# Sums of six weight blocks and of the third row group on VectorE instead of GpSimd, token numbers stored from on-chip rows, a new order of SyncE's transfers, and turn counts loaded at the top of a pair

## The chip, the cores and the metric

The program runs on one core of a Trainium2 chip. The metric is the device time of one execution in microseconds (us); lower is better. Profiles are single executions of the same program, taken by the hardware profiler. In the rows PE is TensorE, DVE VectorE, ACT ScalarE, POOL GpSimd and SP SyncE; an engine's name with a q (DVEq, SPq) is its sequencer, which runs register instructions and issues transfers.

## The reference

The reference chains three blocks on 2304 tokens (4 batches of 576) of width 512. All numbers are float32.

```python
# 1. attention with a feature map, 8 heads of 64; phi(x) = [exp(p), exp(-p)], p = x @ w_phi - max|x @ w_phi|
kv = einsum('bhsf,bhsd->bhfd', phi(k), v); z = sum_s phi(k)
x = (phi(q) @ kv) / (phi(q) @ z + 1e-6)                 # -> (2304, 512)
# 2. mixture of 8 experts, F = 1024, one expert per token
e_idx = argmax(x @ w_gate, axis=1); gate_w = softmax(x @ w_gate)[e_idx]; eom = sigmoid(x @ w_output_gate)
x[mask_e] = gate_w * eom[:, e] * (maximum(x[mask_e] @ w1[e], 0) @ w2[e])
# 3. gated feed-forward block, F = 1536, rms norm ahead of it
xn = x / sqrt(mean(x * x) + 1e-6) * rms_g
out = (silu(xn @ w_gate) * (xn @ w_val)) @ w_out
```

With these inputs three of the eight experts get tokens.

## The kernel before

**Numbers and products.** Each float32 operand of a large product is split into a high part in a reduced format (a copy by ScalarE, names ending in H) and a low remainder (a subtraction by VectorE, names ending in L); three matmuls, high by high, high by low and low by high, replace one. TensorE is busy nearly all the time, so the order of the other engines' work is written out by hand, one program per engine, with semaphores between them. `wait_ge` holds only the engine that issues it, and everything behind it in that engine's program.

**Routing.** Attention's rows, with the token's number in column DM (512) and its gate in column 513, are scattered to `xs_dram`, one region per expert. A table `tab` in SBUF holds, for the active experts in order ("turns"), how many steps each has (TILES), its first step (FIRST), its number, and for each step its row and output column. There are eight steps of 288 rows in this run, 0 to 7, in three turns: steps 0 and 1, steps 2 to 5, and steps 6 and 7. Step 0 is taken early, beside the end of attention. Every engine walks over the table by itself: `over_turns` (on VectorE `turns`) loops over pairs of turns, since weights are double-buffered; for each of the two turns of a pair `turn_of` (L417, L418) loads the number of steps and the first step into registers, and `If(tiles > 0)` skips an empty turn. The fourth turn, the second of the second pair, is empty here.

**A step** has eight chunks m = 0 to 7: hidden(m) and outputs(m - 2) on TensorE, relu and its high half on ScalarE, the low half hmL on VectorE. Beside them, SyncE loads the rows of a step into the one buffer `xin` (`rows_next`, once TensorE has transposed the previous rows, semaphore pe_XT), GpSimd multiplies them by their gates (`gate_rows`), TensorE transposes them at the end of the previous step (L1080), ScalarE copies the step's outputs to `x2g` in the next step's chunk 0 (`copy_out`, L1371; it needs the store of the rows before it to have landed, semaphore xst), GpSimd squares and adds them (`add_squares`), VectorE normalises them (`normal`, L1805), and SyncE stores them to `xn_dram` (`rows_out`). In the first step of a turn the next turn's weights are split, and GpSimd issues their loads (`raw_in`). Each step also prepares the weights of one of the final block's twelve visits: SyncE loads them (`step_weights_in`), VectorE adds (`weight_sums`, L1918 to L1926) and they are split and stored to `t_dram` (`weights_out`). `numbers_out` copies 288 token numbers from `xs_dram` to `ids_dram`, as a transfer of 288 elements of 4 bytes; the numbers are read back once, near the middle of the final block.

**The final block** multiplies by gate and value weights in 2x2 blocks by a scheme of seven products instead of eight, which needs sums of blocks on both sides. A unit is one visit v (128 of 1536 columns of gate and value) for one group sg of 768 rows: seven products of six matmuls each, L1207 to L1209. There are 36 units; UNITS orders them: units 0 to 2 are of group 0, units 3 to 5 of group 1, and group 2 first comes up in unit 10. A group's rows are loaded by `group_in` into `xst`; four sums per group (`row_sums`) go to `s_sum`; ScalarE and VectorE then make seven high and seven low halves. Sums of groups 0 and 2 are made by GpSimd (L863 to L869), of group 1 by VectorE in unit 1 (L2058 to L2068). Visits 6 to 11 (MADE) get their weights raw, and GpSimd makes their sums (`made_sums`, L851 to L855) ahead of MADE_AT; the other visits' operands come from `t_dram` (`operands_in`).

Within unit u VectorE does: first_gate(u), the work listed for position "A", second_gate(u - 1) (L2010, after TensorE's last product of unit u - 1), the work for "B", hidden_rows(u - 1) (L2024 and L2026, after ScalarE's sigmoid, L1482), values(u) (L2018). TensorE's fourth product in unit u + 1, `last_product(u)`, waits for values(u). ScalarE's sigmoid of unit u waits until the hidden rows of unit u - 2, which lie in the same buffer `hid`, are stored (`hidden_out` on SyncE, L640). The outputs follow from h_dram, after 720 us.

**SyncE's order** in the loop over steps and at the entry of the final block is that of its program:

```python
with e.Fori(0, total - 2) as n:
    rows_next(n + 2)          # waits for pe_XT
    weights_out(n + 1)        # waits for the step's split weights
    step_weights_in(n + 2)    # waits until that store has landed
    rows_out(n, col)          # waits for the normalised rows
    numbers_out(n, col, row)
```

## Time and profile before

| | us |
|---|---|
| median of three runs | 870.38 |
| lowest and highest | 868.96, 873.25 |
| the profiled execution, its time | 873.63 |
| its span in the trace | 871.9 |
| TensorE busy | 840.2 |
| VectorE busy | 538.9 |
| ScalarE busy | 347.3 |
| GpSimd busy | 161.4 |

The span is the time from the first to the last instruction of the trace; the profiled execution's own time is 1.7 us more. By stages, attention and step 0 take to 243 us, the steps 1 to 7 to 445 us, the 36 units to 720 us, and the outputs the rest. Matmuls are pipelined, so a matmul's duration is longer than the distance to the next one. A row of waits gives the engine and line that waited, the engine and tile it waited for, the total in us, the number of waits and the longest.

### The profile page before, as it was taken

The page shows a single profiled execution, that of the slowest core. Times are in us where ns is not written, and L with a number is a line of the kernel's source. Part 1 is how long each engine was busy: PE and PEld are TensorE (multiplying, and loading weights), DVE is VectorE, ACT ScalarE, POOL GpSimd, SP SyncE. Part 2 cuts the span into 40 slices and gives each one's busy share as a digit, 9 for nine tenths or more (in the row PEclk, how much of TensorE's full clock was granted, in tenths as well). Part 3 has the DMA queues.
Part 4 walks back from the last instruction along what each step waited for, and adds up shares of the span by engine and source line. Part 5 has one row for each costly group of instructions (what it writes and reads, how often), then busy time and mean ns, then how long its engine had stood idle before and what let it go on. Part 6 is the DMA issues. An engine that isn't in the chain of part 4 may idle for free.

```text
span 871.9 us, 16594 instructions
## 1 busy us (share of the span) xinstructions
PE 840.2 (96%) x6216; PEld 757.3 (87%) x6217; DVE 538.9 (62%) x934; ACT 347.3 (40%) x547; POOL 161.4 (19%) x169
## 2 busy tenths in 40 slices
PE   8999999998988999999989999999999999999997
PEld 6685867767988999999989999999999998888885
DVE  5688786989766954445569777666765774212210
ACT  4544454573155533322354443333433443212211
POOL 1010302112350433203421031111110000101101
PEclk9999999999999999999999999999999999999999
DMA  8613713112349544554662852232421945343320
GB/s 285 209 57 138 275 54 108 55 38 75 127 175 267 227 114 97 141 148 150 184 230 77 280 180 79 79 80 79 142 71 54 357 150 184 123 139 125 125 101 36
DMA packets 65226, 122.41 MB, mean 140 GB/s; under 512 B 9200, under 2 KB 43120, under 8 KB 62480
## 3 DMA queue, kind: packets, MB, share of 16 engines
q1 hardware_dynamic: 57600, 91.98, 34.3%
q0 software_dynamic: 3488, 17.85, 5.3%
q10 hardware_dynamic: 4080, 11.80, 3.9%
...
## 4 chain that ended last, share of the span: by engine, by line
PE 78%; DVE 11%; issue 6%; DMA 2%; ACT 1%; DVEq 1%; SPq 0%; another core or an unknown queue 0%; POOLq 0%; POOL 0%; ACTq 0%
PE ps L1207 9%; PE ps L1209 9%; PE ps L1208 9%; PE ps L1259 5%; PE ps L1258 5%; PE ps L1260 5%; PE ps L956 3%; PE ps L1115 3%; PE ps L1116 3%; PE ps L1117 3%; PE ps L1128 3%; PE ps L1130 3%; PE ps L1129 3%; PE ps L1011 3%; PE ps L916 2%
## 5 line engine op out<-in xcount | busy, mean ns | idle before, releaser
L1207 PE MATMUL ps<-sH,tb 128*128 128x384 f32 x504 | 171.0, 339 | 5.9 <-DVE val L2018 2.9
L1208 PE MATMUL ps<-sL,tb 128*128 128x384 f32 x504 | 170.0, 337 | 0.0
L1209 PE MATMUL ps<-sH,tb 128*128 128x384 f32 x504 | 169.9, 337 | 0.0
L1207 PEld LDWEIGHTS ps<-sH,tb 128*128 128x128 f32 x504 | 95.0, 189 | 8.5 <-DVE val L2018 4.9
L1208 PEld LDWEIGHTS ps<-sL,tb 128*128 128x128 f32 x504 | 95.1, 189 | 0.1
L1209 PEld LDWEIGHTS ps<-sH,tb 128*128 128x128 f32 x504 | 95.2, 189 | 0.0
L2036 DVE TENSOR_TENSOR hTL<-h_st,hTH 128x768 fp32r<-128x768 f32 x36 | 33.0, 954 | 97.4 <-ACT hTH L1516 97.4
L1260 PE MATMUL ps<-woH,hTL 128*128 128x512 f32 x216 | 84.1, 389 | 0.0
L1259 PE MATMUL ps<-woL,hTH 128*128 128x512 f32 x216 | 84.1, 389 | 0.0
L1258 PE MATMUL ps<-woH,hTH 128*128 128x512 f32 x216 | 84.0, 389 | 0.0
L1115 PE MATMUL ps<-xmH,w1H 128*128 128x288 f32 x256 | 76.8, 300 | 5.9 <-issue 2.8
L1128 PE MATMUL ps<-hmH,w2H 128*128 128x288 f32 x256 | 78.7, 307 | 1.8 <-ACT x2g L1371 1.8
L1116 PE MATMUL ps<-xmL,w1H 128*128 128x288 f32 x256 | 76.1, 297 | 0.0
L1117 PE MATMUL ps<-xmH,w1L 128*128 128x288 f32 x256 | 76.0, 297 | 0.0
L1130 PE MATMUL ps<-hmH,w2L 128*128 128x288 f32 x256 | 75.7, 296 | 0.0
L1129 PE MATMUL ps<-hmL,w2H 128*128 128x288 f32 x256 | 75.7, 296 | 0.0
L1784 DVE SCALAR_TENSOR_TENSOR hmL<-ps,hmH 128x288 fp32r<-128x288 f32 x64 | 29.1, 454 | 74.5 <-ACT hmH L1363 73.9
L1363 ACT ACTIVATE hmH<-ps 128x288 fp32r<-128x288 f32 x64 | 26.3, 410 | 95.9 <-PE ps L1130 75.6
L1582 DVE TENSOR_REDUCE mx<-ps 128x4 f32<-128x512 f32 x72 | 49.3, 684 | 20.6 <-PE ps L918 19.4
L1494 ACT ACTIVATE part<-ps 128x384 f32<-128x384 f32 x36 | 17.7, 492 | 109.3 <-PE ps L1209 106.1
L2024 DVE TENSOR_TENSOR hid<-hid,gate 128x768 f32<-128x768 f32 x36 | 35.3, 982 | 38.7 <-ACT hid L1482 38.7
...
## 6 DMA issues: line engine op xcount, KB each, us to landing
...
```

The costliest lines, as they stand in the source:

```text
L1115: e.matmul(o, w1H[par][:, c, cols], xmH[:, c, :], start=(c == 0), stop=False)
L1116: e.matmul(o, w1H[par][:, c, cols], xmL[:, c, :], start=False, stop=False)
L1117: last = e.matmul(o, w1L[par][:, c, cols], xmH[:, c, :], start=False, stop=(c == KC - 1))
L1128: e.matmul(o, w2H[par][:, m, cols], hmH[:, m % 2, :], start=(m == 0), stop=False)
L1129: e.matmul(o, w2H[par][:, m, cols], hmL[:, m % 2, :], start=False, stop=False)
L1130: last = e.matmul(o, w2L[par][:, m, cols], hmH[:, m % 2, :], start=False, stop=(m == FC - 1))
L1207: e.matmul(to, wh, xh, start=(fresh and c == 0), stop=False, skip_group_check=True)
L1208: e.matmul(to, wh, xl, start=False, stop=False, skip_group_check=True)
L1209: done = e.matmul(to, wl, xh, start=False, stop=(c == 1), skip_group_check=True)
L1258: e.matmul(to, hi, woH[:, i, :], start=(i == 0), stop=False, skip_group_check=True)
L1259: e.matmul(to, hi, woL[:, i, :], start=False, stop=False, skip_group_check=True)
L1260: done = e.matmul(to, lo, woH[:, i, :], start=False, stop=(i == NF - 1), skip_group_check=True)
```

## The change

On every engine the loop over a pair of turns loads the counts of both turns first, and the first step (and on VectorE the next count) only inside the branch. Token numbers are stored from column DM of `xin` once the rows of the step are there, and the next load of `xin` waits for that store. In SyncE's loop the rows' store comes ahead of the load of the next step's weights. At the entry of the final block the rows of group 0 are loaded ahead of the operands of visit 0, and those of visit 1 wait for the first high half of group 0 instead of for step 7's hidden chunks. In unit 4 the store of the hidden rows comes behind the load of group 2's rows instead of ahead of the store that this load needs. In a turn's first step GpSimd issues the load of w1 ahead of gating. GpSimd's sums of group 2 and of the six made visits go to VectorE: group 2 at the positions of SUM_AT, a made visit's three sums at position "B" of the unit ahead of MADE_AT. GpSimd keeps the sums of group 0.

```diff
@@ -66,6 +66,8 @@
...
+SUM_AT = {(1, "A"): ((1, 0), (1, 1)), (1, "B"): ((1, 2), (1, 3)), (7, "B"): ((2, 0), (2, 1)), (8, "A"): ((2, 2),),
+          (8, "B"): ((2, 3),)}
...
@@ -412,11 +414,14 @@
...
-        def turn_of(e, x):
-
-            tiles = e.value_load(tab[0:1, bass.ds(x + TILES, 1)], min_val=0, max_val=NTOK // G)
-            first = e.value_load(tab[0:1, bass.ds(x + FIRST, 1)], min_val=0, max_val=NTOK // G + E)
-            return tiles, first
+        def turns_of(e, pair):
+
+            return [e.value_load(tab[0:1, bass.ds(pair * 2 + (par + TILES), 1)], min_val=0, max_val=NTOK // G)
+                    for par in range(2)]
+
+        def first_of(e, x):
+
+            return e.value_load(tab[0:1, bass.ds(x + FIRST, 1)], min_val=0, max_val=NTOK // G + E)
...
@@ -432,9 +437,10 @@
...
             with e.Fori(0, pairs) as pair:
-                for par in range(2):
-                    tiles, first = turn_of(e, pair * 2 + par)
+                counts = turns_of(e, pair)
+                for par, tiles in enumerate(counts):
                     with e.If(tiles > 0):
+                        first = first_of(e, pair * 2 + par)
                         if once is not None:
                             once(pair, par)
...
@@ -533,6 +539,16 @@
...
+            def numbers_out(n, col):
+
+                e.wait_ge(s["ld"], n * 16 + 16)
+                settle(e, "carry_sp")
+                e.wait_ge(s["idst"], n * 16 + 16)
+                settle(e, "carry_sp")
+                with nc.allow_non_contiguous_dma(reason="token numbers"):
+                    e.dma_start(ids_dram[bass.ds(col, G), :].rearrange("(t p) a -> p t a", p=GR), xin[:, :, DM:DM + 1])\
+                        .then_inc(s["idst"], 16)
+
...
@@ -550,7 +566,9 @@
...
                 rows_in(x0 * REGION)
+                numbers_out(0, 0)
                 e.wait_ge(s["pe_XT"], KC)
+                e.wait_ge(s["idst"], 32)
                 rows_in(x0 * REGION + G)
...
@@ -576,15 +594,9 @@
                 row = row_of(n)
                 e.wait_ge(s["pe_XT"], n * KC)
                 settle(e, "carry_sp")
-                rows_in(row)
-
-            def numbers_out(n, col, row):
-
                 e.wait_ge(s["idst"], n * 16 + 16)
                 settle(e, "carry_sp")
-                with nc.allow_non_contiguous_dma(reason="token numbers"):
-                    e.dma_start(ids_dram[bass.ds(col, G), :], xs_dram[bass.ds(row, G), DM:DM + 1])\
-                        .then_inc(s["idst"], 16)
+                rows_in(row)
...
@@ -604,17 +616,18 @@
...
                 weights_out(0)
                 step_weights_in(1)
+            numbers_out(1, column_of(1))
             with e.Fori(0, total - 2) as n:
                 rows_next(n + 2)
                 weights_out(n + 1)
+                numbers_out(n + 2, column_of(n + 2))
+                rows_out(n, column_of(n))
                 step_weights_in(n + 2)
-                col, row = column_of(n), row_of(n)
-                rows_out(n, col)
-                numbers_out(n, col, row)
             rows_next(total)
...
@@ -652,37 +665,31 @@
...
             e.wait_ge(s["pe_s1"], last * FC + 1)
             settle(e, "carry_sp")
-            e.wait_ge(s["e_st"], 16 * 8)
-            operands_in(0)
             e.wait_ge(s["xst"], total * 16)
             settle(e, "carry_sp")
             group_in(0)
-            prior_col, prior_row = column_of(prior), row_of(prior)
-            rows_out(prior, prior_col)
-            e.wait_ge(s["pe_s1"], total * FC)
-            settle(e, "carry_sp")
+            e.wait_ge(s["e_st"], 16 * 8)
+            operands_in(0)
+            rows_out(prior, column_of(prior))
+            e.wait_ge(s["s_hi0"], 1)
             operands_in(1)
             e.wait_ge(s["pe_s2"], total * FC + 2)
             settle(e, "carry_sp")
             group_in(1)
             e.wait_ge(s["s_lo"], 5)
             operands_in(2)
-            last_col, last_row = column_of(last), row_of(last)
+            last_col = column_of(last)
             for u in range(NU):
-                hidden_out(u)
                 if u == ROOT_AT + 1:
                     rows_out(last, last_col)
                     e.wait_ge(s["s_lo"], 7)
                     e.wait_ge(s["xst"], total * 16 + 32)
                     settle(e, "carry_sp")
                     group_in(2)
+                hidden_out(u)
                 for vis in MADE:
                     if last_of_visit(vis - 3) == u + 1:
                         weights_in(vis)
-                if u == 8:
-                    numbers_out(prior, prior_col, prior_row)
-                if u == 10:
-                    numbers_out(last, last_col, last_row)
...
@@ -827,9 +834,10 @@
...
             def split_step(pair, par, g):
                 add_squares(g - 1)
+                with e.If(has_turn(pair * 2 + (par + 2))):
+                    raw_in(1, pair * 2 + (par + 2), pair * (2 * PIECES) + ((par + 1) * PIECES + KC))
                 gate_rows(g + 1)
                 with e.If(has_turn(pair * 2 + (par + 2))):
-                    raw_in(1, pair * 2 + (par + 2), pair * (2 * PIECES) + ((par + 1) * PIECES + KC))
                     raw_in(2, pair * 2 + (par + 2), pair * (2 * PIECES) + (par + 2) * PIECES)
...
@@ -844,42 +852,26 @@
...
-            def made_sums(v):
-
-                n, st = nth_made(v), t_raw[v % 3]
-                e.wait_ge(s[f"w_in{v % 3}"], 16 * (n // 3) + 16)
...
-            def row_sums(sg, half):
-
-                x, to = xst[sg], s_sum[sg]
-                done = 4 * (sg // 2)
...
             total = total_steps(e)
-            row_sums(0, 0)
+            row_sums(0)
             e.wait_ge(s["e_lo"], total)
             settle(e, "carry_pool")
-            row_sums(0, 1)
+            row_sums(1)
             e.wait_ge(s["s_lo"], 7)
             add_squares(total - 1)
-            e.wait_ge(s["s_lo"], 14)
-            row_sums(2, 0)
-            row_sums(2, 1)
-            for vis in MADE:
-                made_sums(vis)
             e.wait_ge(s["id_c"], 1)
...
@@ -1962,11 +1954,12 @@
...
                 with e.Fori(0, pairs) as pair:
-                    for par in range(2):
-                        tiles, first = turn_of(e, pair * 2 + par)
-                        nxt = e.value_load(tab[0:1, bass.ds(pair * 2 + (par + TILES + 1), 1)], min_val=0,
-                                           max_val=NTOK // G)
+                    counts = turns_of(e, pair)
+                    for par, tiles in enumerate(counts):
                         with e.If(tiles > 0):
+                            first = first_of(e, pair * 2 + par)
+                            nxt = e.value_load(tab[0:1, bass.ds(pair * 2 + (par + TILES + 1), 1)], min_val=0,
+                                               max_val=NTOK // G)
                             with e.Fori(0, tiles) as t:
                                 step(pair, par, first + t, nxt - t * (NTOK // G))
...
@@ -2038,9 +2041,13 @@
...
             def beside(u, pos):
 
+                for sg, n in SUM_AT.get((u, pos), ()):
+                    row_sum(sg, n)
                 for sg, o in LOW_AT.get((u, pos), ()):
                     row_low(sg, o)
                 for vis in MADE:
+                    if (u, pos) == (MADE_AT[vis] - 1, "B"):
+                        made_sums(vis)
...
@@ -2050,22 +2057,20 @@
...
-            def row_sums(n):
...
+            def row_sum(sg, n):
+
+                x, to, done = xst[sg], s_sum[sg], s[f"s_add{sg}"]
                 if n == 0:
-                    e.wait_ge(s["x_in1"], 16)
-                    e.tensor_tensor(to[5][:, :, :], x[:, 0:2, GN:2 * GN], x[:, 2:4, GN:2 * GN], ALU.add).then_inc(s["s_add1"], 1)
-                    return
+                    e.wait_ge(s[f"x_in{sg}"], 16)
+                    e.tensor_tensor(to[5][:, :, :], x[:, 0:2, GN:2 * GN], x[:, 2:4, GN:2 * GN], ALU.add).then_inc(done, 1)
...
@@ -2080,15 +2085,9 @@
             for u in range(1, NU):
                 first_gate(u)
                 beside(u, "A")
-                if u == 1:
-                    row_sums(0)
-                    row_sums(1)
                 if u == ROOT_AT:
                     mean(total - 1, BANKS[u % 2][3])
                 second_gate(u - 1)
-                if u == 1:
-                    row_sums(2)
-                    row_sums(3)
                 beside(u, "B")
...
```

`row_sum(sg, n)` on VectorE is the old `row_sums(n)` for any group, and `sums_done` follows the new semaphores s_add0 to s_add2, one per group. SyncE waits for s_add2 instead of s_add ahead of the load of the output weights in unit 20.

## Rows read from the trace of the kernel before

**Rows 1.** the page, section 1, share of the span.

```profile
PE 840.2 (96%) x6216; PEld 757.3 (87%) x6217; DVE 538.9 (62%) x934; ACT 347.3 (40%) x547; POOL 161.4 (19%) x169
```

**Rows 2.** waits of TensorE, 205 to 310 us: total, times, longest.

```profile
PE ps L1115 <- issue: 2.3, 2, 1.6
PE ps L1128 <- ACT x2g L1371: 1.8, 1, 1.8
```

**Rows 3.** waits of TensorE, 430 to 470 us.

```profile
PE ps L1207 <- DVE sL L1998: 2.5, 1, 2.5
```

**Rows 4.** waits of TensorE, 470 us to the end.

```profile
PE ps L1207 <- DVE val L2018: 2.3, 5, 1.5
```

**Rows 5.** chain that ended last, 441 to 449 us: start, duration, what.

```profile
442.92 0.81 DVEq L417
...
444.90 0.31 DVEq L1967
...
446.80 0.97 DVE sL L1998
```

**Rows 6.** busy time by stretch, 448 to 452 us; PEclk before the last two.

```profile
448.00:452.00 4.00, 4.00 (x15) 4.00 (x15) 2.60 (x4) 3.12 (x5) 0.00 (x0) 0.58 1.02 410
```

**Rows 7.** timeline of SyncE's queue, 440 to 447 us.

```profile
441.43 1.68 SPq L624 DMA_DIRECT2D tb<-t_dram  x2
```

**Rows 8.** tile xst, the load issued at 445.39 us.

```profile
DMA to landing us min/median/max: 8.0/8.0/8.0
```

**Rows 9.** timeline of VectorE, 458 to 459 us.

```profile
458.50 0.95 DVE L2058 TENSOR_TENSOR s_sum<-xst 128x768 f32<-128x768 f32 x1
```

**Rows 10.** chain that ended last, 272 to 284 us.

```profile
271.01 9.75 DMA xn_dram<-x2g
```

**Rows 11.** timeline of VectorE, 264 to 270 us.

```profile
265.48 1.79 DVE L1805 SCALAR_TENSOR_TENSOR x2g<-x2g,gcol,rinv 128x288 f32<-128x288 f32 x4
```

**Rows 12.** tensor ids_dram, its eight stores and the read.

```profile
DMA to landing us min/median/max: 3.7/8.1/9.1
```

**Rows 13.** tile xin, its nine loads.

```profile
DMA to landing us min/median/max: 4.4/9.3/10.5
```

**Rows 14.** timeline of GpSimd, 254 to 262 us.

```profile
254.42 6.77 POOL L779 TENSOR_SCALAR xin<-xin 96x512 f32<-96x512 f32 x3
```

**Rows 15.** timeline of TensorE, 266 to 270.5 us.

```profile
267.76 0.66 PE L1080 MATMUL ps<-ident,xin 96*128 96x96 f32 x6
```

**Rows 16.** timeline of VectorE, 503 to 522 us.

```profile
506.24 0.56 DVE L2010 TENSOR_TENSOR gate<-part,ps 128x384 f32<-128x384 f32 x1 [1.50 <-PE ps L1209]
508.54 0.96 DVE L2024 TENSOR_TENSOR hid<-hid,gate 128x768 f32<-128x768 f32 x1 [1.75 <-ACT hid L1482]
...
510.59 0.96 DVE L2018 TENSOR_TENSOR val<-ps,part 128x768 f32<-128x768 f32 x1
...
513.51 0.55 DVE L2010 TENSOR_TENSOR gate<-part,ps 128x384 f32<-128x384 f32 x1 [1.50 <-PE ps L1209]
...
520.25 0.96 DVE L2018 TENSOR_TENSOR val<-ps,part 128x768 f32<-128x768 f32 x1
```

**Rows 17.** timeline of GpSimd, 505 to 520 us.

```profile
510.51 1.86 POOL L863 TENSOR_TENSOR s_sum<-xst 128x768 f32<-128x768 f32 x1 [48.29 <-DMA xst<-xn_dram]
```

**Rows 18.** timeline of VectorE, 277 to 280 us.

```profile
277.88 0.68 DVE L1918 TENSOR_TENSOR t_raw<-t_raw 128x512 f32<-128x512 f32 x1
...
279.28 0.42 DVE L1926 TENSOR_TENSOR t_raw<-t_raw 128x256 f32<-128x256 f32 x1
```

**Rows 19.** timeline of VectorE, 491 to 495 us.

```profile
492.06 1.80 DVE L1805 SCALAR_TENSOR_TENSOR x2g<-x2g,gcol,rinv 128x288 f32<-128x288 f32 x4
```

**Rows 20.** timeline of SyncE's queue, 490 to 505 us.

```profile
496.85 0.65 SPq L593 DMA_DIRECT2D xn_dram<-x2g  x1
503.33 0.57 SPq L635 DMA_DIRECT2D xst<-xn_dram  x1
```

**Rows 21.** tensor h_dram, the store issued at 503.96 us.

```profile
DMA to landing us min/median/max: 9.2/9.2/9.2
```

50 lines of the change are left out of this document (27 added, 23 removed).

## The prediction

> **What bounds the kernel now.** I began with the busy shares: TensorE works 840.2 of 871.9 us [rows 1]. So nothing that makes another engine cheaper pays by itself; only the 32 us in which TensorE does nothing, and any stretch of slower clock, can be won. The table of TensorE's waits, stage by stage, says what can be reached. In the expert stage the reader is to see 2.3 us under "issue" (the entries of two turns: register loads, no semaphore) and 1.8 us in one wait for ScalarE's copy x2g [rows 2]. At the entry of the final block it waits 2.5 us for the first low half of the rows, sL [rows 3]. From 470 us on it waits 2.3 us in five pieces for VectorE's val, the longest 1.5 us [rows 4]. These are the places that the change can touch; attention (before 205 us) and the last 150 us it leaves as they are.
>
> **The change part by part.**
>
> **Entry of the final block.** The chain there runs through VectorE's sequencer: three loads from the table, the first at 442.92 and the last at 444.90, then the copy of the first high half and sL at 446.80 [rows 5]. They are the loads for the fourth turn, which has no steps. After the edit its count is loaded at the top of the pair, and its first and next are only loaded inside the branch. That is 2.3 us, near 2.6 with their bookkeeping, and ScalarE loses two loads of the same kind. sL starts at 444.2 instead of 446.8 and ends near 445.2; TensorE's last matmul before the wait ends at 446.8 + 1.0 - 2.5 = 445.3. The wait of 2.5 us goes whole. Behind it the granted clock is 0.58 in the mean of 448 to 452 us [rows 6], that is 1.2 GHz for (1 - 0.58) / 0.5 = 84% of 4 us, 3.4 us, of which half is lost: 1.7 us. The wait of 1.8 us [rows 2] drew no such stretch, so without the longer one I count it as won. Sum -4.2.
>
> Something is given back. SyncE now holds the load of the second visit's operands for the first high half (s_hi0): issue near 444.2 instead of 441.43 [rows 7], with the load of group 1's rows, still held to 445.4 by the outputs, behind them. Those took 8.0 us, to 453.4 [rows 8]; with the operands' 1.75 MB 2.8 us later ahead of them I put them at 455.4, while VectorE, which took them up at 458.50 [rows 9], would now be there 4 us earlier, at 454.5. Bounds 0 (the load is early enough) and 2.5 us (the whole shift reaches the path through VectorE's two dependent sums). I take 0.7. Net -3.5.
>
> **SyncE's order in the expert stage.** ScalarE's copy x2g waited for the store of the previous step's rows, issued at 271.01 and 9.75 us under way [rows 10]. Ahead of it on the queue stands the load of the next step's weights, which waits for the store of the step's own to land. The rows were normalised at 265.48 + 1.79 = 267.3 [rows 11]. In the new order the store goes out at 267.4, 3.6 us earlier, with the token numbers 5 us ahead of it rather than behind. ScalarE wants it about 2 us before 280.8: the wait of 1.8 us goes, bounds 0 and 1.8. Sum -1.8.
>
> **Token numbers from the rows on chip.** The same eight stores of 1.1 KB, each 8.1 us in the median [rows 12], now read xin, and each must land before xin is loaded again. For steps 2 and later it is issued in mid step and its landing is hidden by the rest of the step. For step 1 it is issued near 239 and the load of step 2's rows, 240.59 before, waits for it: to 247.5 at 8.1 us, to 253 if it starts only after the weights under way on the same engines. Loads of xin took 4.4 to 10.5 us [rows 13]; they ran right behind a numbers store in all but the early ones, which no longer happens. The rows land at 252 to 260. GpSimd, which gated them from 254.42 in 6.8 us beside VectorE's work [rows 14], now does so by 267 at the latest; the transposes want them at 267.76 [rows 15]. Cost 0, with 1 us to spare at worst. GpSimd also issues w1's load before it gates; that load starts 2 us earlier and its reader is a whole turn away: 0. The stores of numbers at units 8 and 10 fall away, hidden anyway: 0.
>
> **Turn entries.** A load with its bookkeeping takes about 0.7 us of a sequencer: the first and third of the three stand 1.98 apart, the first being 0.5 longer than usual [rows 5]. TensorE's entries of turns 0 and 2 (even places in the pair) now have three loads ahead of the first matmul instead of two: +0.7 each. Turn 1 has one instead of two: -0.7. Net +0.7; bounds 0 (hidden behind queued matmuls) and +1.5.
>
> **Sums moved to VectorE.** The row view of a unit gives the room. second_gate starts at 506.24, the product with the gate at 508.54, val at 510.59, and the next second_gate at 513.51, 7.3 us on [rows 16]. Before the product VectorE is idle for 1.8 us while ScalarE makes the sigmoid. With GpSimd's sums running, from 510.51 on [rows 17], val came at 520.25, 2.4 us after its turn of 517.9 [rows 16]; TensorE idled 1.5, so it tolerates 0.7 to 0.9 us of lateness. All four later waits coincide with GpSimd's sums; without them the 2.3 us [rows 4] go. One visit's three weight sums took VectorE 277.88 to 279.70, 1.8 us [rows 18]: they fit the gap. Only at unit 22 they come on top of a low half of 1024 elements (0.96 x 4/3 = 1.3 us): 1.3 + 1.8 - 1.8 - 0.8 = 0.5; bounds 0 and 1. Group 2's sums are 0.96 each, two in the gap of unit 7, one ahead of second_gate in unit 8 (1.5 us idle there) and one in its gap: 0. Sum -2.3 + 0.5 = -1.8.
>
> **The store of unit 4's hidden rows.** This is where I expect a new wait. It moves behind the load of group 2's rows. The last rows are normalised at 492.06 + 1.80 = 493.9 [rows 19]; their store goes out there instead of at 496.85, and the group load, which waits for it, followed at 503.33 [rows 20]. ScalarE's queue has 1.75 MB of operands under way at that time, so I take the group load only 1.6 us earlier (bounds 0 and 2.8): 501.7. It landed 7.1 us after its issue (510.5, rows 17): 508.8. A hidden store issued just behind it took 9.2 us, to 513.2 [rows 21], 2.7 us after the rows. Unit 4's store is in that place now: landing 510.4 to 511.5, I take 510.8. ScalarE's sigmoid of unit 6 writes the same buffer and waits for it. It would have started 0.88 us ahead of 508.54, at 507.66; it starts 3.1 us late, everything behind it (0.88 us to the product, 3.0 more to val's end) too, and after 0.7 us of tolerance TensorE waits 2.4 us in unit 8. VectorE's own wait for the rows in unit 7 (508.8 + 1.9 = 510.7) ends before that. Bounds 0 and 3.7.
>
> **The sum.** -3.5 - 1.8 + 0.7 - 1.8 + 2.4 = -4.0 us. The profiled execution took 873.63 us (span 871.9); it would take 869.6. It stood 3.25 above the median of the three runs, 870.38, so I forecast 866.4 as the median. A measurement of this kernel tells about 0.5%, 4.35 us, from no change (its three runs spread over 4.3): the forecast lies on that bound.
>
> **The rivals.**
>
> No new wait in unit 8. If the stores from SyncE's queue share the engines with ScalarE's loads instead of standing behind them, the last rows are stored by 499.5, the group load lands at 506.6 and unit 4's store at 509.2: sigmoid 1.5 us late, 0.8 us at TensorE, total 864.8. For it: both queues use the same sixteen engines. Against it: the rows' store, issued at 496.85, landed only just ahead of 503.33, some 6.4 us later [rows 20]. Chance 0.2. The Trainium skill, DMA: Bandwidth & Descriptors, section Queues, rings and completion order, says that an engine round-robins between the queues that have work, packet by packet; by that rule this rival is the likelier, and the trace's 6.4 us speak for waiting.
>
> The clock falls again. The wait of 2.4 us in unit 8, or the entry of turn 1's pair (1.6 + 0.7 = 2.3), is close to the 2.5 us behind which the clock fell [rows 3, 6]; another 1.7 us each: 868 to 870, no change. Chance 0.15.
>
> The gain at the entry of the final block is given back. Group 1's rows, late by the queue, hold VectorE at its sums, then the sigmoid of unit 0 and val of unit 1: +2.5 instead of +0.7 and the clock still at half for want of work: 869. Chance 0.12.
>
> Slower. The numbers store of step 1 decides. It starts behind 4 MB of weights, and eight stores of 1.1 KB needing 8 to 9 us each are slow already [rows 12]. If it lands later than 256.6, 17 us after its issue, then with 4.4 for the load and 6.8 for the gating the transposes are late, and TensorE stalls one for one. At 26 us the stall has eaten the 4.0 and 4.35 more: a median of 874.7. Chance 0.06.
>
> **How the numbers follow.** The forecast case has 0.47, with a range of its own of 863 to 869 from the bounds above, half of it on either side of 866.0. Faster by over 0.5%: 0.26 from it, 0.2 from the first rival, 0.02 of others: 0.48. Slower by over 0.5%: 0.06. The rest, 0.46, is no change. The range that leaves out 1 in 10 on each side is 861.5 to 870.5.
>
> **What would show it.** Right: no wait of TensorE for sL above 0.5 us at the block's entry and a clock of 1.00 from 444 to 452; no wait for x2g near 280; GpSimd without a sum after 440 except the squares; VectorE's products 0.96 us throughout; a TensorE wait of 1.5 to 3 us for val in unit 8, with ScalarE's sigmoid waiting for h_dram; waits under "issue" of 2.3 and 1.3 us at the entries of turns 0 and 2 and near 0 at turn 1. Wrong: a landing of group 2's rows before 507; a store of numbers over 14 us; a wait of TensorE for xmL or for gated rows near 268; product gaps of over 1.8 us on VectorE in units 12 to 25.

## The result

| us | before | after |
|---|---|---|
| median | 869.74 | 880.57 |
| lowest and highest, four runs each | 868.96, 873.25 | 878.78, 881.68 |
| the profiled execution, its time | 873.63 | 881.11 |
| its span | 871.9 | 879.5 |

The ratio of the times is 1.0115, with a 95% interval of 1.0081 to 1.0148: the change makes the kernel 10.8 us slower, where 4.0 us less (866.4) were forecast. The page of after, section 1, busy time and share (compare [rows 1]):

```profile
PE 842.6 (96%) x6216; PEld 762.6 (87%) x6217; DVE 541.7 (62%) x956; ACT 347.5 (40%) x547; POOL 127.0 (14%) x147
```

VectorE's busy time grew by 2.8 us net and GpSimd's fell by 34; TensorE's work is the same to 2.4 us, part of which is a slower clock. So the time went into waits. The waits of TensorE of after, 205 to 310 us: total, times, longest (compare [rows 2]):

```profile
PE ps L1107 <- DVE hmL L1776: 6.2, 2, 5.5
PE ps L1120 <- ACT x2g L1363: 3.5, 1, 3.5
PE ps L1107 <- issue: 2.3, 1, 2.3
```

From 430 to 470 us [rows 3] there is one of 1.4 us for ScalarE's copy part. And from 470 us to the end [rows 4]:

```profile
PE ps L1199 <- DVE val L2021: 6.8, 3, 6.2
```

The wait for sL is gone. One of 5.5 us for hmL and one of 6.2 us for val are new, and the wait for x2g, which was to go, grew from 1.8 to 3.5. The clock was at half behind both. Busy time by stretch of after; PEclk is the column before the last two:

```profile
276.00:280.00 4.00, 1.26 (x10) 0.93 0.93 288
280.00:284.00 4.00, 3.23 (x12) 0.50 0.97 371
284.00:288.00 4.00, 0.02 (x1) 0.50 0.53 121
288.00:292.00 4.00, 2.48 (x10) 0.50 0.00 0
```

The same around unit 8:

```profile
516.00:520.00 4.00, 0.00 (x0) 0.80 0.03 8
520.00:524.00 4.00, 3.03 (x9) 0.50 0.34 98
524.00:528.00 4.00, 4.00 (x21) 0.85 0.00 0
```

From 280 to 292 the granted clock is 0.50, which is 1.2 of 2.4 GHz, behind four microseconds in which TensorE worked 1.26; around 520 the same, for (0.20 + 0.50 + 0.15) x 4 / 0.5 = 6.8 us.

**By stages.** The distance from the first matmul of one stage to that of the next, read from TensorE's timeline, shows where the time went. Step 2 to step 3, for example, was 275.16 to 306.64 before and is 272.20 to 311.99 after. Differences to the profiled execution of before, for after and the runs below (us):

| stretch | after | e0 | e1 | e2 | e3 | e4 | e5 | e6 | e7 |
|---|---|---|---|---|---|---|---|---|---|
| step 0 to 1 | 2.3 | 0.0 | 0.8 | 0.9 | 0.0 | 0.8 | 0.0 | 0.8 | 0.0 |
| step 1 to 2 | 0.4 | 0.1 | -0.3 | -0.4 | -0.8 | 0.6 | 0.0 | -0.8 | -0.4 |
| **step 2 to 3** | **8.3** | 0.4 | 3.0 | 8.8 | 9.4 | 0.8 | 0.7 | -2.2 | -2.3 |
| step 3 to 7 | 1.0 | 0.7 | 1.0 | 1.0 | 1.6 | 1.5 | 0.1 | 1.0 | 0.2 |
| step 7 to unit 0 | -3.4 | 0.7 | -3.4 | -3.4 | -2.6 | 0.0 | 0.8 | -3.4 | -0.1 |
| unit 0 to 3 | -0.7 | 0.0 | -0.8 | -0.9 | -0.7 | -1.7 | -0.1 | 0.4 | -0.9 |
| **unit 8 to 9** | **8.5** | 0.0 | 8.0 | 3.3 | 7.4 | 0.0 | 4.6 | 6.9 | 0.8 |
| unit 9 to 10 | -1.8 | 0.0 | -1.8 | -1.8 | -1.8 | 0.0 | -1.8 | -1.8 | -1.8 |
| unit 12 to 30 | -1.3 | -1.0 | -1.3 | -1.3 | -1.3 | -0.8 | -1.3 | -1.3 | -1.3 |

| stretch | e8 | e9 | e10 | e11 | e12 | e13 | e14 | e15 |
|---|---|---|---|---|---|---|---|---|
| step 0 to 1 | 0.0 | 1.5 | 0.1 | 0.0 | 1.5 | 1.5 | 2.3 | 1.5 |
| step 1 to 2 | 0.1 | -0.6 | -0.5 | -0.5 | -0.6 | -0.8 | -0.8 | -0.5 |
| **step 2 to 3** | 0.1 | -2.4 | -2.4 | -2.4 | -2.3 | -2.3 | 2.3 | -2.4 |
| step 3 to 7 | 0.5 | 0.2 | 0.3 | 0.2 | 0.2 | 0.2 | 14.9 | 0.2 |
| step 7 to unit 0 | -1.2 | -1.3 | -2.6 | -2.6 | -2.6 | -2.6 | 1.3 | -2.6 |
| unit 0 to 3 | 0.6 | -0.7 | -1.5 | -0.8 | -1.5 | -1.6 | -0.4 | -1.6 |
| **unit 8 to 9** | 0.0 | 0.0 | 3.4 | 0.8 | 7.6 | 0.0 | 6.0 | 0.0 |
| unit 9 to 10 | 2.0 | -1.8 | -1.0 | -1.8 | -1.8 | -1.8 | -1.8 | -1.8 |
| unit 12 to 30 | 0.7 | -1.3 | -1.3 | -1.3 | -1.3 | -1.3 | -1.3 | -1.3 |

The rest of a profile differs by up to 5.7 us in attention, which no edit touches: e0, the kernel before again, started step 0 2.0 us later than the first profile of it, and after 5.6 us earlier. It goes with the chip of a group of runs: step 0 starts at 216.7 to 219.5 us in e0 to e3, 215.8 to 217.4 in e4 to e7 and 210.5 to 211.0 in e8 to e15. So a part is judged by its own stretch, and the medians judge whole kernels. For after the stretches add up to +13.3; with the 5.6 us of attention the span is 7.6 longer, and the medians, of several executions each, say 10.8. Unit 12 to 30 moved by 1.0 in e0 too; a difference under 1 us there says nothing. One profile can also differ from another by a wait that the edits don't explain: e9 and e11 have the same program up to unit 4 and stand 1.3 us apart in step 7 to unit 0.

**The first two rows of after.** The +2.3 of step 0 to 1 are 0.8 for the entry of step 1 and 1.5 for a half clock at the start of step 0, behind a wait of 2.0 us for xmL there. Busy time by stretch of after:

```profile
212.00:216.00 4.00, 4.00 (x23) 0.67 0.03 6
```

The same stands in the profiles of e9 and e12 to e15, behind waits of 1.9 to 2.1 us, and not in e8, e10 and e11, behind 1.8 to 2.1. The wait is the same in e8, which differs from before at the entry of the final block alone, so the change did not make these 1.5 us. The entry of step 1, now 2.3 us long, has a half clock of its own behind it:

```profile
240.00:244.00 4.00, 2.17 (x9) 0.74 0.82 331
244.00:248.00 4.00, 4.00 (x28) 0.83 0.06 4
```

This one lies in step 1 to 2, which is +0.4 instead of the -0.8 of e6.

**Step 2 to 3 of after.** The chain of work that ended last, 256 to 292 us: start, duration, what.

```profile
258.71 18.70 DMA t_dram<-tb
...
277.65 9.48 DMA t_raw<-in_ffn_up
...
287.26 0.70 DVE t_raw L1910
```

SyncE's queue, 255 to 290 us: start, length of the issue, line, transfer.

```profile
258.71 0.37 SPq L612 DMA_DIRECT2D t_dram<-tb  x1
260.07 0.34 SPq L549 DMA_DIRECT2D ids_dram<-xin  x1
265.36 0.70 SPq L605 DMA_DIRECT2D xn_dram<-x2g  x1
277.65 0.37 SPq L579 DMA_DIRECT2D t_raw<-in_ffn_up  x1
279.46 0.34 SPq L553 DMA_DIRECT2D xin<-xs_dram  x1
```

GpSimd's timeline in the same stretch:

```profile
257.54 0.58 POOL L825 DMA_DIRECT2D w1raw<-in_w  x1 [5.08 <-issue]
```

(DMA_DIRECT2D is the issue of a transfer.) w1's load goes out 1.2 us ahead of the store of the step's split weights, and that store takes 18.70 us. The next weights' load must wait for it (277.65), takes 9.48 more, and VectorE, which works in order, stands at these weights' sums until 287.26 while TensorE wants hmL, queued behind them. The numbers (260.07) and the rows' store (265.36) lie in the same pile: the rows took 14.1 us to land, 9.75 before [rows 10], so x2g was late too. The sixteen DMA engines were not idle meanwhile: SyncE's queue moved 0.44 MB from 270 to 277 us of after in 84% of their time, and 1.14 MB from 299 to 306 us of before in 56%, where the next weights' load and the rows' store lie ahead of the numbers. (w2's load on GpSimd's queue begins in after's seven microseconds too, so not all of it is the numbers' doing.)

**Unit 8 of after.** VectorE's timeline; in brackets the idle time before and what ended it (compare [rows 16]):

```profile
508.51 0.55 DVE L2013 TENSOR_TENSOR gate<-part,ps 128x384 f32<-128x384 f32 x1 [1.50 <-PE ps L1201]
514.44 0.96 DVE L2065 TENSOR_TENSOR s_sum<-xst 128x768 f32<-128x768 f32 x1 [5.37 <-DMA xst<-xn_dram]
...
517.90 0.96 DVE L2027 TENSOR_TENSOR hid<-hid,gate 128x768 f32<-128x768 f32 x1 [1.51 <-ACT hid L1474]
...
519.96 0.96 DVE L2021 TENSOR_TENSOR val<-ps,part 128x768 f32<-128x768 f32 x1
```

ScalarE's timeline:

```profile
517.02 0.84 ACT L1474 ACTIVATE hid<-gate 128x768 f32<-128x768 f32 x1 [6.98 <-DMA h_dram<-hid]
```

SyncE's queue (compare [rows 20]):

```profile
496.38 0.63 SPq L605 DMA_DIRECT2D xn_dram<-x2g  x1
506.17 0.57 SPq L648 DMA_DIRECT2D xst<-xn_dram  x1
506.79 13.45 SPq L653 DMA_DIRECT2D h_dram<-hid  x3
```

Two waits lie in parallel. VectorE stands at the sums of group 2 until the rows have landed (514.4), and ScalarE's sigmoid until the hidden rows of unit 4 are stored (516.94). val ends at 520.9; TensorE had wanted it 6.2 us earlier.

### The profile page after: what moved, and what is told of

It is laid out like the page before. It is cut to its first block, busy times and chain, and to the rows that moved or that the text cites. A ratio compares the mean times of both kernels' runs of the same rounds, so it can differ in the third digit from the quotient of the medians.

```text
span 879.5 us, 16574 instructions
## 1 busy us (share of the span) xinstructions
PE 842.6 (96%) x6216; PEld 762.6 (87%) x6217; DVE 541.7 (62%) x956; ACT 347.5 (40%) x547; POOL 127.0 (14%) x147
## 4 chain that ended last, share of the span: by engine, by line
PE 79%; DVE 8%; DMA 7%; issue 4%; ACT 1%; SPq 0%; DVEq 0%; POOLq 0%; POOL 0%; ACTq 0%
PE ps L1199 9%; PE ps L1200 9%; PE ps L1201 9%; PE ps L1252 5%; PE ps L1250 5%; PE ps L1251 5%; PE ps L1107 4%; PE ps L1108 3%; PE ps L1109 3%; PE ps L1120 3%; PE ps L1121 3%; PE ps L1122 3%; PE ps L948 3%; PE ps L1003 3%; DMA t_dram<-tb 2%
## 5 line engine op out<-in xcount | busy, mean ns | idle before, releaser
L1107 PE MATMUL ps<-xmH,w1H 128*128 128x288 f32 x256 | 78.9, 308 | 11.8 <-DVE hmL L1776 6.2
L1108 PE MATMUL ps<-xmL,w1H 128*128 128x288 f32 x256 | 78.1, 305 | 0.0
L1109 PE MATMUL ps<-xmH,w1L 128*128 128x288 f32 x256 | 77.8, 304 | 0.0
L1107 PEld LDWEIGHTS ps<-xmH,w1H 128*128 128x128 f32 x256 | 50.0, 195 | 14.1 <-DVE hmL L1776 7.7
```

What stands on the lines that cost most here:

```text
L1107: e.matmul(o, w1H[par][:, c, cols], xmH[:, c, :], start=(c == 0), stop=False)
L1108: e.matmul(o, w1H[par][:, c, cols], xmL[:, c, :], start=False, stop=False)
L1109: last = e.matmul(o, w1L[par][:, c, cols], xmH[:, c, :], start=False, stop=(c == KC - 1))
```

## The experiments

Each group of four ran on one chip, and each kernel is compared with the kernel before on its chip (medians 876.29, 876.23, 871.44 and 870.73 us). All kernels compute the whole reference. Ratios are to before, with their 95% intervals. The kernel after was not run again in these groups, so a run is compared with it by its stretches, or through the two ratios.

### e0 to e3: the kernel before again, and three edits of after

> The kernel before once more, for a second profile of it. The profiled execution of before reached step 0 at 216.25 us and that of the changed kernel at 210.64, though the change leaves attention alone. If the 5.6 us are chance of the single execution (transfers that arrive early or late in three places), the second profile will stand elsewhere in attention while all stages behind it agree within 0.5 us. If it is again at 216, the change speeds attention in a way that was not seen. Time 870 +- 3.

> The changed kernel with one part undone: in a turn's first step GpSimd gates the rows first and issues w1's load behind, as before. Theory A: the extra 8.3 us of step 2 come from w1's load, issued at 257.54 and now 1.2 us ahead of the store t_dram instead of 0.3 us behind it; then t_dram lands in about 8 us instead of 18.7, TensorE's wait of 5.5 us for hmL and the one of 3.5 us for x2g near 281 go, the clock stays at 1.00 from 279 to 293, and the median falls by 7 to 9 us, to 872 to 874. Theory B: they come from the token numbers' store of 4-byte elements that now stands in front of the rows' store; then the rows' store still takes over 12 us, a wait for x2g of 2 to 4 us stays and the median falls by less than 4.

```diff
 def split_step(pair, par, g):          # GpSimd, e1: as in the kernel before
     add_squares(g - 1)
-    with e.If(has_turn(...)): raw_in(1, ...)      # w1
     gate_rows(g + 1)
+    with e.If(has_turn(...)): raw_in(1, ...)
```

> The changed kernel with one part undone: unit 4's hidden rows are stored ahead of the last rows' store and of group 2's load, as before. Theory: the extra 8.5 us of unit 8 are ScalarE's sigmoid of unit 6 waiting for that store; TensorE's wait of 6.2 us for val goes wholly, and with it the 6.8 us at half clock; group 2's rows then land later than VectorE wants them for its sums in unit 7, which costs 0.5 to 2 us there. Median lower by 6 to 8 us, 872.5 to 874.5. Rival: the sums moved to VectorE make the wait, since VectorE stands at group 2's rows ahead of the products; then a wait of over 4 us stays in unit 8.

```diff
 for u in range(NU):                    # SyncE, e2
+    hidden_out(u)
     if u == ROOT_AT + 1:
         rows_out(last, last_col)
         ...
         group_in(2)
-    hidden_out(u)
```

> The changed kernel with the counts of the two turns loaded one by one again, each ahead of its own branch, while the first step and VectorE's next count stay inside the branch. Two loads instead of three at the entries of turns 0 and 2, one load more than now at the end of the stage. Theory: TensorE's waits under issue at these two entries fall by 0.75 us each (2.3 to 1.6 and 1.3 to 0.5), the half clock behind the first of them, 3.4 us from 241.9, goes (1.7 us), and VectorE reaches the first high half about 0.7 us later than now. Median lower by 2 to 3 us. Rival: the clock's fall there has nothing to do with the length of this wait; then 1.5 us and no more.

```diff
-counts = turns_of(e, pair)             # every engine, e3
-for par, tiles in enumerate(counts):
+for par in range(2):
+    tiles = tiles_of(e, pair * 2 + par)
     with e.If(tiles > 0):
```

Measured: e0 876.68 (ratio 1.001, 0.9992 to 1.0029). e1 879.40 (1.003, 1.0005 to 1.0055): w1's load behind gating gives back 5.3 of the 8.3 us of step 2 to 3. The whole kernel gained what theory A asked, but the waits of theory B stayed: the rows' store still takes 12.7 us. e2 885.28 (1.0107, 1.0059 to 1.0155): the store first gives back 5.1 of the 8.5 us of unit 8. 3.3 stay, and there VectorE waits for group 2's rows. The 6 to 8 us expected of the whole kernel are not in its ratio, which is after's 1.0115 within the noise; why is open. e3 886.52 (1.0123, 1.0091 to 1.0155): the counts one by one take the 0.8 us from the turns' entries and give up 0.8 of the gain at unit 0. The entry of step 1 is 1.6 us again and no half clock follows, as the theory said; the 2 to 3 us expected of the whole kernel don't show in its ratio. The waits of TensorE in e1, 205 to 310 us, show what is left in step 2, beside 2.1 us for x2g:

```profile
PE ps L1106 <- DVE hmL L1775: 3.1, 1, 3.1
```

### e4 to e7: parts of the change on the kernel before, and a combination

> The kernel before with one part of the change: counts of both turns loaded at the top of the pair, first step and next count inside the branch, on all engines. Theory: this part alone makes three of the differences: TensorE's stall at the start of step 1 grows by 0.8 us and the half clock behind it adds 1.7 (interval step 0 to step 1 +2.3), step 5 to 6 +0.8, and the entry of the final block (step 7 to unit 0) -3.4. Sum near 0 (-0.3), nothing else moves. Rival: the entry of the block is gained by SyncE's new order there (rows of group 0 first, operands of visit 1 held), then step 7 to unit 0 stays within 0.5 of before and this kernel is 3 us slower.

```diff
-        tiles, first = turn_of(e, pair * 2 + par)      # e4: the hunks of turns_of and first_of of the change, all engines
+counts = turns_of(e, pair)
```

> The kernel before with one part of the change: the sums of group 2 and of the six made visits on VectorE, at the same positions; SyncE's order in unit 4 stays as before. Theory H: VectorE at position B of unit 7 waits for the rows of group 2, which land near 510.4; values of unit 7 end 4.9 us after the landing (as in the run with the store first), at 515.3, where TensorE wants them at 512.3: wait of 3.0 us in unit 8, interval unit 8 to 9 +3 to +5 with the clock behind it; then unit 9 to 10 -1.8 and unit 12 to 30 -1.3 (GpSimd's sums no longer slow VectorE). Sum 0 to +2. Rival: unit 4's late store makes the whole wait of unit 8; then unit 8 to 9 within 0.5 of before, sum -3.1.

```diff
+SUM_AT = {..., (7, "B"): ((2, 0), (2, 1)), (8, "A"): ((2, 2),), (8, "B"): ((2, 3),)}   # e5: the hunks of SUM_AT,
-            for vis in MADE: made_sums(vis)            # row_sums and made_sums of the change, SyncE as before
```

> The changed kernel with w1's load behind gating again, and the token numbers copied from xs_dram as before, issued last in SyncE's loop; the rows' store still ahead of the load of the next step's weights. With w1's load alone behind gating, step 2 to 3 was still 3.0 us longer than before. Theory B: the store of 4-byte elements ahead of the rows' store makes both late (8 to 12 us each); without it step 2 to 3 is at or below before: -1.8 to +0.5, and no wait of TensorE for hmL there. Rival: the load of the step's weights, now behind the rows' store, is late by itself and VectorE waits for it: step 2 to 3 stays +2 to +3. Total: 3 us less than the run with w1's load behind gating by theory B, the same by the rival.

```diff
 with e.Fori(0, total - 2) as n:        # SyncE, e6 against after; w1's load is behind gating too, as in e1
     rows_next(n + 2)
     weights_out(n + 1)
-    numbers_out(n + 2, column_of(n + 2))      # from xin
     rows_out(n, col)
     step_weights_in(n + 2)
+    numbers_out(n, col, row)                  # from xs_dram
```

> The kernel before with the parts that gained: counts loaded one per turn with first and next inside the branch (entry of the final block -2.6, no cost at turn entries); sums of group 2 and of the made visits on VectorE, but those of group 2 half a unit later (first two at unit 8 A, third at 8 B, fourth at 9 A, ScalarE's high half that needs it at 9 C), so that VectorE does not wait for rows that land at 510.4; the rows' store ahead of the load of the next step's weights, numbers last and from xs_dram as before. Expected if the parts add up: -2.6 (entry), -0.7 (units 0 to 3), -1.8 (unit 9 to 10), -1.3 (units 12 to 30), 0 to -1.8 (wait for x2g): -6.4 to -8.2 us, ratio 0.991 to 0.993. If the rows' load of group 2 is still waited for in unit 8: -3, ratio 0.996.

```diff
+SUM_AT = {..., (8, "A"): ((2, 0), (2, 1)), (8, "B"): ((2, 2),), (9, "A"): ((2, 3),)}   # e7
-(9, "A"): ((2, 2), (2, 3), (2, 4)), (9, "C"): ((2, 5),)       # HIGH_AT
+(9, "A"): ((2, 2), (2, 3)), (9, "C"): ((2, 4), (2, 5))
```

e7 has e5 with this SUM_AT, e4 with the counts one by one as in e3, and the loop of e6.

**e4**: 875.08 (0.9986, 0.9964 to 1.0009). The entries cost 0.8 as expected, but the interval step 7 to unit 0 did not move. Against the theory sL's wait went and another took its place. VectorE's timeline of e4 in step 7:

```profile
438.09 6.91 DVE L1809 SCALAR_TENSOR_TENSOR x2g<-x2g,gcol,rinv 128x288 f32<-128x288 f32 x4
```

GpSimd's in the same stretch:

```profile
438.74 1.93 POOL L869 TENSOR_TENSOR s_sum<-s_sum,xst 128x768 f32<-128x768 f32 x1
440.75 1.93 POOL L872 TENSOR_TENSOR s_sum<-xst,s_sum 128x768 f32<-128x768 f32 x1
```

The four instructions that normalise the rows took 6.91 us, beside GpSimd's sums of group 0; with no such neighbour they take 1.79 together [rows 11]. The low half xmL behind them is late and TensorE waits 1.8 us for it. Busy time by stretch of e4 behind that wait:

```profile
444.00:448.00 4.00, 2.24 (x14) 0.84 0.37 128
448.00:452.00 4.00, 4.00 (x24) 0.73 1.01 315
```

That is (0.16 + 0.27) x 4 / 0.5 = 3.4 us of half clock. Whether it is contention, e8 tests.

**e5**: 876.99 (1.0017, 0.9996 to 1.0038). VectorE's timeline of e5 in unit 7, with the old order of SyncE (val is done at 517.7, and TensorE had wanted it 2.7 us earlier):

```profile
512.79 0.96 DVE L2058 TENSOR_TENSOR s_sum<-xst 128x768 f32<-128x768 f32 x1 [3.45 <-DMA xst<-xn_dram]
...
516.71 0.96 DVE L2014 TENSOR_TENSOR val<-ps,part 128x768 f32<-128x768 f32 x1
```

The sums wait 3.45 us for the rows and unit 8 to 9 is 4.6 us longer: theory H holds without the late store. The gains behind it are as forecast: unit 9 to 10 -1.8.

**e6**: 874.20 (0.9977, 0.9955 to 0.9998). Step 2 to 3 goes from +3.0 (e1) to -2.2: theory B. The load of the next weights, 290 to 420 us, shows what the numbers' place does. From issue to landing, before, with the numbers behind it:

```profile
DMA to landing us min/median/max: 3.1/3.2/3.3
```

After, with the numbers and the rows' store ahead of it:

```profile
DMA to landing us min/median/max: 8.3/8.4/8.9
```

In e6, with only the rows' store ahead of it, the three are 4.2, 4.8 and 8.8. The landing of the rows' store, 295 to 415 us, in before (numbers issued 1.1 us behind it) and in e6 (1.8 us behind it):

```profile
DMA to landing us min/median/max: 3.5/6.6/9.0
DMA to landing us min/median/max: 3.7/3.8/3.9
```

So the numbers also delay the transfer just ahead of them when they follow it closely. e6 differs from e1 in their source (xs_dram instead of xin) as well as in their place; no run separates the two, but the numbers of before come from xs_dram too, and they delayed the rows' store.

**e7**: 866.81 (0.9889, 0.9864 to 0.9914), somewhat more than the sum expected. Unit 8 to 9 is +0.8, so the late sums cost little here. Step 7 to unit 0 has gained nothing: VectorE waited 1.0 us there for t_raw.

### e8 to e11: the entry of the final block

> The kernel before with one part of the change: SyncE's order at the entry of the final block (rows of group 0 loaded ahead of the operands of visit 0, operands of visit 1 held for the first high half). The counts at the turns stay as before. The register loads of the fourth turn alone, taken away in an earlier run, removed the wait for sL but the interval step 7 to unit 0 stayed (-0.02): TensorE waited 1.8 us for xmL instead, because VectorE's normalising ran beside GpSimd's sums of group 0 at 2.08 us an instruction instead of 0.5. Theory C (contention): with group 0 loaded first GpSimd's sums end about 1.5 us earlier and fewer of the four instructions are long; no wait for xmL, but the wait for sL stays at 2.5: step 7 to unit 0 -0.5 to -1.5. Rival: the order alone brings the -3.4.

```diff
-e.wait_ge(s["e_st"], 16 * 8); operands_in(0)                 # SyncE, e8: as in after
 e.wait_ge(s["xst"], total * 16); group_in(0)
+e.wait_ge(s["e_st"], 16 * 8); operands_in(0)
 rows_out(prior, prior_col)
-e.wait_ge(s["pe_s1"], total * FC)
+e.wait_ge(s["s_hi0"], 1)
 operands_in(1)
```

> The combined kernel (counts inside the branch, late sums of group 2 on VectorE, rows' store first, numbers last) with the changed kernel's order at the entry of the final block: rows of group 0 ahead of the operands of visit 0, those of visit 1 held for the first high half. In the combined kernel VectorE waited 1.0 us for t_raw in step 7, whose load shared the queue with the operands, and all four normalising instructions ended 2.8 us later than before. Expected: step 7 to unit 0 -2.6 to -3.4 instead of -0.1, unit 0 to 3 between -0.7 and +0.4 instead of -0.9; in all 2 to 3 us less than the combined kernel: ratio to before 0.985 to 0.987. Rival: the order at the entry gives nothing by itself, ratio 0.989 as before.

e9 is e7 with the diff of e8.

> The same, but the operands of visit 1 wait for step 7's hidden chunks, as in the kernel before, instead of for the first high half. Theory: the hold costs 0.4 to 1.5 us, since ScalarE's copies of unit 0 and the rows of group 1 came late (TensorE waited 1.8 us for part in the run with the old numbers store); without it the wait for part in unit 0 falls below 1 us. Rival: the hold keeps the queue free for the rows of group 0 and its loss costs as much; no difference within 0.5 us.

```diff
-e.wait_ge(s["s_hi0"], 1)               # SyncE, e10 against e9
+e.wait_ge(s["pe_s1"], total * FC)
 operands_in(1)
```

> As the run with rows of group 0 first, and in unit 4 the last rows' store is issued ahead of unit 4's hidden rows, whose store still comes ahead of the load of group 2. Expected: that store goes out about 3 us earlier and the rows of group 2 land 1 to 3 us earlier (the load waits for the store); the wait in unit 8 goes (interval unit 8 to 9 from +0.8 to 0). Rival: the hidden store, now behind the rows' store, lands late and ScalarE's sigmoid of unit 6 waits for it: unit 8 to 9 +1 or more.

```diff
 for u in range(NU):                    # SyncE, e11
+    if u == ROOT_AT + 1:
+        rows_out(last, last_col)
     hidden_out(u)
     if u == ROOT_AT + 1:
-        rows_out(last, last_col)
```

**e8**: 870.98 (0.9989, 0.9968 to 1.0011). Step 7 to unit 0 -1.2, the wait for sL still 2.2 and none for xmL: theory C. GpSimd's sums end earlier, and the four normalising instructions, here VectorE's row of e8, take half as long as in e4:

```profile
430.31 3.30 DVE L1804 SCALAR_TENSOR_TENSOR x2g<-x2g,gcol,rinv 128x288 f32<-128x288 f32 x4
```

The two edits of the entry give 0.0 and -1.2 alone and -3.4 together (after, e1, e2, e6, which hold other edits too): each had been covered by what the other takes away. The 2.0 us that e8 lost in unit 9 are mostly clock: TensorE waits 1.9 us for val there, and the granted clock behind it is 0.68 and 0.89 from 516 to 524 us, 1.00 in before. **e9**: 860.88 (0.9886, 0.9862 to 0.9910): no gain over e7's ratio, which is the rival. Its stretch from step 7 to unit 0 gained 1.2 us on e7's, with a wait of 1.3 us for hmL in step 7 that e10 and e11 don't have; its +1.5 in step 0 to 1 is the half clock at the start of step 0. The normalising is back to 2.15 us for four.

**e10**: 858.09 (0.9857, 0.9832 to 0.9883), 13.4 us under before, the lowest ratio, though its interval overlaps those of e9, e11, e13 and e15. The hold for s_hi0 cost 0.8 us in units 0 to 3 (also e11 against e15). Its profiled run took 862.4 us, while its other four runs took 857.8 to 858.2, and the trace shows why. Group 2's rows landed at 502.60, 4.7 us after the start of unit 8 (0.9 in e13), and ScalarE stood before them with TensorE's next copy part behind:

```profile
502.62 1.58 ACT L1465 ACTIVATE sH<-xst 128x768 fp32r<-128x768 f32 x2 [4.03 <-DMA xst<-xn_dram]
```

VectorE's first late sum waited 2.9 us for the same rows, TensorE 2.4 for part, and the clock fell behind it (0.87 and 0.70 from 504 to 512 us). So the late sums are free only while these rows land in time. **e11**: 859.82 (0.9881, 0.9855 to 0.9907): no measurable gain from the last rows' store ahead, and unit 8 to 9 is +0.8, not the 0 expected.

### e12 to e15: single edits put back into the fastest kernel

> The combined kernel with rows of group 0 first and no hold of visit 1's operands (late sums of group 2, so that VectorE does not wait for its rows), with one edit of the change put back: in unit 4 the store of the hidden rows comes behind the load of group 2's rows. This measures by itself the term that was forecast at 2.4 us (bounds 0 to 3.7). Theory: the store took 5.1 of the 8.5 us of unit 8 (what the run with it first gave back), so unit 8 to 9 is 4 to 6 us longer than in the kernel without this edit, with ScalarE's sigmoid of unit 6 waiting for h_dram. Rival: with VectorE's wait for the rows gone the store's landing is hidden in part: +1 to +3, as forecast.

> The same combined kernel with another edit of the change put back alone: GpSimd issues w1's load ahead of gating in a turn's first step. Token numbers are here copied last and from xs_dram, the rows' store ahead of the next weights' load. Theory: w1's load ahead of the step's own store on the sixteen engines makes that store late by 9 to 12 us, and the next weights behind it, whatever the numbers do: step 2 to 3 +5 us over the kernel without the edit (-2.35 to about +3). Rival: it was the pile of w1 and the stores of 4 bytes together; alone it costs under 1.5 us.

> The changed kernel with w1's load behind gating, and the token numbers still stored from the rows on chip, but behind the rows' store instead of ahead of it (still ahead of the load of the next step's weights). With the store ahead step 2 to 3 was +2.95 against before, with numbers last and from xs_dram -2.2. Theory Q: it is the place that costs, since what is issued behind a store of 4-byte elements takes 8 to 13 us instead of 5 to 8; the rows' store is then as fast as with numbers last, but the load of the weights is still behind it: step 2 to 3 between -1 and +2.5, with VectorE waiting for t_raw. Rival: the delay comes from the store of rows and weights colliding, not from the numbers: step 2 to 3 stays at +2.95.

> The combined kernel with rows of group 0 first, no hold of visit 1's operands, and the last rows' store ahead of unit 4's hidden rows. Removing the hold gave 1 to 3 us, the last rows' store first 0 to 1. If they add up: 0.982 to 0.986 of before. Rival: the earlier store of the last rows makes the hidden store late: no better than without it, 0.986.

e12 and e13 are e10 with the diffs of e2 and e1 turned round, e15 is e10 with that of e11, and e14 is e1 with this:

```diff
     weights_out(n + 1)                 # SyncE, e14 against e1
-    numbers_out(n + 2, column_of(n + 2))
     rows_out(n, column_of(n))
+    numbers_out(n + 2, column_of(n + 2))
     step_weights_in(n + 2)
```

**e12**: 866.52 (0.9953, 0.9934 to 0.9972). Unit 8 to 9 is +7.6 where e13 and e15, with the same units, have 0.0. ScalarE's timeline in unit 8:

```profile
502.21 0.84 ACT L1471 ACTIVATE hid<-gate 128x768 f32<-128x768 f32 x1 [5.25 <-DMA h_dram<-hid]
```

TensorE waits 4.5 us for val there. So the store alone costs 4.5 us of waiting and some 3 of slow clock (0.67 and 0.50 from 504 to 512 us): the theory, and more than it asked.

**e13**: 859.77 (0.9877, 0.9854 to 0.9899). Step 2 to 3 is -2.3, as without the edit: the rival. The store of the split weights did become slower, if by less than the theory's 9 to 12 us. Its landing in e13, 252 to 282 us (8.0 in e10):

```profile
DMA to landing us min/median/max: 12.6/12.6/12.6
```

But the load of the next weights behind it then took 3.2 instead of 8.3 us, and VectorE took them up at 272.98, hardly later than in e10 (271.90). So w1's load costs nothing alone; with the numbers' store in the pile (e1 against after) it costs 5.3.

**e14**: 890.84 (1.0247, 1.0218 to 1.0277), the slowest of all. Step 2 to 3 is +2.3, as theory Q allowed, but neither theory saw that steps 3 to 7 together get 14.9 us longer than before (e1: 1.0). TensorE's waits, 300 to 440 us:

```profile
PE ps L1106 <- DVE hmL L1775: 14.0, 5, 3.3
```

The chain that ended last, 300 to 336 us:

```profile
299.96 10.11 DMA t_raw<-in_ffn_up
...
329.44 10.48 DMA t_raw<-in_ffn_up
```

The landing of the weights' loads, 290 to 440 us:

```profile
DMA to landing us min/median/max: 10.1/10.5/11.3
```

The weights' load, issued 0.7 us behind the numbers' store, takes 10.5 us in the median instead of 3.2 (8.4 in after, where it cost nothing in these steps), and it is now on the path in every step. The rows' store, 1.6 us ahead of the numbers, took 5.5 to 6.9 us there, not the 3.8 of numbers last. **e15**: 860.24 (0.9879, 0.9862 to 0.9897), not told apart from e10 or e13: the two gains did not add up.

## Why the prediction was wrong

**Entry of the final block, -3.5: the size right, the cause half right.** Step 7 to unit 0 and on to unit 3 gave -3.4 and -0.7, the wait for sL went, and the clock stayed high, as the stretch of after shows (compare [rows 6]):

```profile
448.00:452.00 4.00, 3.94 (x28) 1.00 0.20 35
```

But the working gave all of it to the register loads; those alone (e4) give 1.7 in the two stretches, because VectorE's normalising, slowed by GpSimd's sums, was late next. SyncE's order, in which I had only seen something given back, was the other half. What its hold gives back was right: 0.8 in units 0 to 3 (e9 against e10) for the 0.7 forecast.

**SyncE's order in the expert stage, -1.8: right by itself, overrun in after.** With the numbers out of the way the rows' store ahead of the weights gives -2.2 to -2.4 in step 2 to 3 (e6, e7). I had put the late landing of the rows' store down to the weights' load ahead of it; the numbers 1.1 us behind it had a part in it as well. In after the wait for x2g grew instead.

**Token numbers, 0: the first step that failed.** I followed the store of numbers to its one reader, the next load of xin, and that part was right (step 1's landed after 13.5 us, xin at 254.1, and GpSimd gated it from 258.2). I did not cost what stands behind it on SyncE's queue: the rows' store and the next weights. That is 5.1 us in step 2 to 3 (e1 against e6, source and place together), and 13.9 us over steps 3 to 7 where the weights stand right behind it (e14 against e1, the place alone). The store at 260.07 took 18.7 us to land, over the 14 that the prediction had named as a sign of being wrong. In the kernel before the numbers came last, and the only transfer behind them was the load of xin, which has half a step to spare. [rows 13] already had the price: the loads of xin, nearly all right behind a numbers store, took 9.3 us in the median and 4.4 at the least.

**w1's load ahead of gating, 0: right alone (e13), wrong in this company.** With the numbers in the pile it made the step's own store take 18.7 us, 5.3 us of the 8.3. I had asked for its reader and not for what it delays. The Trainium skill, DMA: Bandwidth & Descriptors, section Queues, rings and completion order, says that an engine takes the queues in turn, packet by packet; the trace of e13 agrees in part only. w1's load, on GpSimd's queue q0, was issued at 255.42 and the store at 256.58. Packets, MB and share of the engines' time, first from 258.5 to 261 us (q0 alone), then from 261 to 264.5:

```profile
q0 software_dynamic: 52, 0.85, 96.6%
...
q0 software_dynamic: 43, 0.70, 50.7%
q1 hardware_dynamic: 48, 0.69, 45.9%
```

From 261 us on the two shared about evenly, but until then the store moved no packet, 4.4 us after its issue. In e10, with the store issued 0.3 us ahead of w1's load, it moved 127 packets up to 261 us and w1's load none. So which of two large transfers is issued first decided here which waits.

**Turn entries, +0.7: right, but not what followed the first** (+0.8, -0.8, +0.8 in e6 at steps 1, 2 and 6). The rival "the clock falls again" had named this entry, at 2.3 us, with a chance of 0.15. It came: behind entries of 2.3 to 2.4 us the clock fell to half in after, e1, e2 and e4, and not in e6 and e14; behind entries of 1.6 us it fell in none of the twelve other profiles. Busy time by stretch just behind that entry, in e1 and then in e6:

```profile
248.00:252.00 4.00, 4.00 (x20) 0.62 0.41 145
248.00:252.00 4.00, 4.00 (x32) 1.00 0.71 171
```

Step 1 to 2 is 0.4 to 1.4 us longer with it (e2 and e4 against e6); the rival had 1.7. What decides between e1 and e6 the runs don't tell.

**Sums on VectorE, -1.8: the gain right, group 2 wrong.** The products stayed at 0.96 us, unit 9 to 10 gave 1.8, unit 22 showed nothing. "VectorE's own wait for the rows in unit 7 ends before that" failed: the sums at position B of unit 7 wait 3.45 us for the rows in e5, where SyncE's order is that of before, and unit 8 to 9 is 3.3 to 4.6 us longer without the late store, slow clock included (e2, e5). The working had these rows land at 508.8, some 1.6 us earlier than in before, and had the wait covered by the sigmoid's. Half a unit later the sums cost 0.0 to 0.8 us (e9, e7), and more when the rows are late (e10).

**The store of unit 4's hidden rows, +2.4: the mechanism right, the size wrong.** It is 7.6 by itself (e12), beyond the bound of 3.7. The last rows' store, ahead of all this, took 9.7 us where I had 7.8, and the hidden store 10.2 where I had 8.5 ([rows 21] had said 9.2). With the issues between, the landing was 3.9 us later than forecast, which is what the wait of 6.2 has over 2.4. The rest is the clock, which I had made a rival instead of a consequence of a stall that long. The other rival for this place, no new wait because the queues share the engines, is refuted by the same 9.7 us.

Of the rivals, the slower one named the right transfer with the wrong victim: it priced the numbers store by xin and the gated rows, which were never late.

**What is left open.** Why the clock fell behind the entry of step 1 in e1 and not in e6, and behind the wait ahead of step 0 in e9 and not in e8; why e2's median kept so little of its stretch's gain; whether the numbers' source has a part beside their place; why group 2's rows came late in e10's profiled run; and which of e10, e13 and e15 is best.
